# Attention, gated MLP and routed experts on one core: VectorE's row transpose moved into a PSUM bank, and another order of the first expert tiles while the last chunk is routed

## What is computed

```python
scores = scale * q @ k.T, causal window of 64, softmax        # 4 x 8 heads, 576 positions, 64 wide
x = attention output as 2304 tokens x 512
xn = x / rms(x) * rms_g
x = (silu(xn @ w_gate) * (xn @ w_val)) @ w_out                # 512 -> 1536 -> 512
logits = x @ w_gate2;  noisy = logits + log1p(exp(x @ w_noise)) * noise   # 8 experts
top-2 experts per token, softmax weights over the two
out[token] += weight * (relu(x[token] @ w1[e]) @ w2[e])       # 512 -> 1024 -> 512
```

## Time and profile before

| | |
|---|---|
| median of three executions | 1112.79 us (1111.0 to 1114.4) |
| profiled execution, its own time | 1109.55 us |
| its span, first to last instruction | 1107.7 us |
| mean granted TensorE clock | 0.995 |
| TensorE matmul busy | 1076.5 us, 97% of the span |
| VectorE busy | 587.5 us, 53% |
| ScalarE busy | 324.2 us, 29% |
| GpSimd busy | 404.6 us, 37% |

### The profile page before, as it was taken

One profiled execution on the slowest core, in us unless ns is written; L12 is line 12 of the kernel. 1 busy time (PEld: TensorE's weight loads), 2 busy tenths in 40 slices (PEclk: granted clock), 3 DMA queues, 4 the chain that ended last, 5 costly groups with the idle time before them and its releaser, 6 DMA issues.

```text
span 1107.7 us, 20151 instructions
## 1 busy us (share of the span) xinstructions
PE 1076.5 (97%) x6113; PEld 940.3 (85%) x6114; DVE 587.5 (53%) x1209; ACT 324.2 (29%) x712; POOL 404.6 (37%) x370
## 2 busy tenths in 40 slices
PE   8999999999999999999998899999999999999995
PEld 7878999999998999999986788888888888888884
DVE  6777334353352353453447767565655666565551
ACT  7996122332431432432353002030302020110241
POOL 3557992022022022010187107070706142331485
PEclk9999999999999999999999999999999999999998
DMA  7975527013013022010185427171625353332675
GB/s 213 270 243 194 171 86 276 1 58 114 1 59 115 1 74 80 5 54 1 46 245 172 110 48 199 38 199 47 179 65 153 78 134 110 99 90 52 172 231 190
DMA packets 167356, 129.40 MB, mean 117 GB/s; under 512 B 96720, under 2 KB 128864, under 8 KB 167296
## 3 DMA queue, kind: packets, MB, share of 16 engines
q1 hardware_dynamic: 145440, 71.20, 22.9%
q10 hardware_dynamic: 16032, 38.47, 11.0%
q0 software_dynamic: 5824, 18.95, 5.1%
HBM read 85.87 MB, written 42.73 MB: 116 GB/s over the span
## 4 chain that ended last, share of the span: by engine, by line
PE 87%; POOL 4%; issue 3%; DMA 2%; DVE 2%; ACT 1%; SPq 0%; POOLq 0%; ACTq 0%; DVEq 0%
PE bank L792 26%; PE bank L953 18%; PE bank L969 18%; PE bank L824 13%; PE bank L982 3%; PE bank L738 3%; PE bank L765 2%; POOL token_rows_a L679 1%; PE bank L748 1%; PE bank L732 1%; PE bank L860 1%; DMA token_rows_b<-expert_rows,slots_u 1%; POOL token_rows_a L692 1%; ACT p_sb L1102 1%; PE bank L871 1%
## 5 line engine op out<-in xcount | busy, mean ns | idle before, releaser
L792 PE MATMUL bank<-x_parts,mlp_weights 128*128 128x384 f32 x1704 | 311.9, 337 | 0.4 <-issue 0.4
L792 PEld LDWEIGHTS bank<-x_parts,mlp_weights 128*128 128x128 f32 x1704 | 296.9, 188 | 6.1 <-issue 0.8
L953 PE MATMUL bank<-expert_parts,xT_high 128*128 (+1 forms) x688 | 217.2, 397 | 6.2 <-DVE xT_low L1640 5.4
L969 PE MATMUL bank<-expert_parts,hT_high 128*128 (+1 forms) x688 | 212.0, 389 | 1.5 <-DVE hT_low L1651 1.5
L663 POOL TENSOR_TENSOR expert_parts<-raw_expert_a,expert_parts 128x512 fp32r<-128x512 f32 x64 | 82.1, 1315 | 243.9 <-ACT expert_parts L1249 243.9
L824 PE MATMUL bank<-mlp_weights,hidden_parts 128*128 128x512 f32 x648 | 162.2, 394 | 1.1 <-ACT y_sb L1173 1.1
L953 PEld LDWEIGHTS bank<-expert_parts,xT_high 128*128 128x128 f32 x688 | 126.6, 189 | 31.4 <-issue 4.7
L969 PEld LDWEIGHTS bank<-expert_parts,hT_high 128*128 128x128 f32 x688 | 129.0, 188 | 28.3 <-issue 1.7
L824 PEld LDWEIGHTS bank<-mlp_weights,hidden_parts 128*128 128x128 f32 x648 | 120.0, 188 | 24.9 <-ACT y_sb L1173 1.4
L953 PE MATMUL bank<-expert_parts,xT_low 128*128 (+1 forms) x344 | 134.8, 392 | 0.0
L969 PE MATMUL bank<-expert_parts,hT_low 128*128 (+1 forms) x344 | 134.1, 390 | 0.0
(11 more groups left out here) (204 smaller groups left out, 1238.6 us busy)
## 6 DMA issues: line engine op xcount, KB each, us to landing
raw_expert_a<-in_w ACTq DMA_DIRECT2D x32, 512.0 KB, 4.0
raw_expert_b<-in_w ACTq DMA_DIRECT2D x32, 512.0 KB, 4.4
x_row<-routed_rows SPq DMA_DIRECT2D x172, 64.0 KB, 2.6
expert_rows<-y_row SPq DMA_DIRECT2D x43, 256.0 KB, 2.0
expert_rows<-zeros SPq DMA_DIRECT2D x4, 2304.0 KB, 13.0
v_sb<-in_v SPq DMA_DIRECT2D x32, 256.0 KB, 3.6
q_sb<-in_qT SPq DMA_DIRECT2D x16, 288.0 KB, 3.7
k_sb<-in_kT SPq DMA_DIRECT2D x16, 288.0 KB, 4.2
```

Of the source, the lines that this page charges most:

```text
L792: last = nc.tensor.matmul(bank[:, 0:CHUNK], w_sb[:, i, wp, at:at + P], xp[:, par, part, k, :], start=n == 0, stop=n == 3 * KB - 1)
L953: last = nc.tensor.matmul(ps[half][:, 0:512], (xTh, xTl)[xp][:, k, :], ew_sb[:, bass.ds(slot, 1), wp, k * F2 + half * 512:k * F2 + half * ...
L969: last = nc.tensor.matmul(ps[5][:, 0:D], (hTh, hTl)[hp][:, f, :], ew_sb[:, bass.ds(slot, 1), 2 + wp, f * D:(f + 1) * D].rearrange("p a n - ...
```

## The change

It has two parts. First, `x_T` is no longer an SBUF tensor but bank 6 of PSUM, for all 43 tiles, so the block transpose writes PSUM, and the rounded copy and the subtraction read PSUM. Second, the opening order changes. On TensorE, the logits product of the last chunk goes between the two halves of the k loop of tile 0's second up half; tile 1's first up half goes ahead of `pe_hT(0)`; the counts and ranks go into the middle of tile 1's second up half; `pe_hT(1)` and tile 2's first up half go ahead of the table's rows. On VectorE, `dve_xT` is cut in three, and its parts for tile 1 stand around the copies of the logits; ReLU of tile 0's second half comes after them; `dve_top2` comes ahead of `dve_hT(0)`, and `dve_slots` stands between the two halves of `dve_hT(0)`, ahead of ReLU of tile 1.

```diff
--- before.py
+++ after.py
@@ -195,7 +195,6 @@
     assert moe.pos - keep.pos <= KB * CHUNK * 8
     xTh = moe.take("xT_high", [P, KB, P], F32R)
     xTl = moe.take("xT_low", [P, KB, P], F32R)
-    x_T = moe.take("x_transposed", [P, KB, P], F32)
     relu = moe.take("relu", [P, F2], F32)
     hTh = moe.take("hT_high", [P, FB2, P], F32R)
     hTl = moe.take("hT_low", [P, FB2, P], F32R)
@@ -940,7 +939,8 @@
             mlp_loop(pe, pe_chunk)
             pe_down(pe, CHUNKS - 1, FB - 1)
 
-        def pe_up2(pe, t, slot, expert, halves=(0, 1)):
+        def pe_up2(pe, t, slot, expert, halves=(0, 1), between=None):
+
             pe.wait_ge(xTl_done, t + 1)
 
             pe.wait_ge(expert_low, 16 * expert + 8)
@@ -949,6 +949,8 @@
                     pe.wait_ge(relu_done, 2 * t - 1 + half)
                 n = 0
                 for k in range(KB):
+                    if between and half == halves[-1] and k == KB // 2:
+                        between()
                     for wp, xp in PRODUCTS:
                         last = nc.tensor.matmul(ps[half][:, 0:512], (xTh, xTl)[xp][:, k, :],
                                                 ew_sb[:, bass.ds(slot, 1), wp, k * F2 + half * 512:k * F2 + half * 512 + 512].rearrange("p a n -> p (a n)"),
@@ -990,19 +992,22 @@
             pe_up2(pe, 0, 0, 0, (0,))
             for t in range(CHUNK_TILES):
                 pe_yT(pe, c, t)
-            pe_up2(pe, 0, 0, 0, (1,))
-            pe_logitsT(pe, c)
+            pe_up2(pe, 0, 0, 0, (1,), lambda: pe_logitsT(pe, c))
             pe_logits(pe, c)
+            pe_up2(pe, 1, 0, 0, (0,))
             pe_hT(pe, 0)
-            pe_up2(pe, 1, 0, 0)
-            pe.wait_ge(chosen_done, CHUNKS)
-            pe_chunk_counts(pe)
-            pe_count(pe, counted)
-            pe_ranks(pe, c)
+
+            def ranks():
+                pe.wait_ge(chosen_done, CHUNKS)
+                pe_chunk_counts(pe)
+                pe_count(pe, counted)
+                pe_ranks(pe, c)
+            pe_up2(pe, 1, 0, 0, (1,), ranks)
             pe_down2(pe, 0, 0, 0)
+            pe_hT(pe, 1)
+            pe_up2(pe, 2, 0, 0, (0,))
             pe_table_rows(pe)
-            pe_hT(pe, 1)
-            pe_up2(pe, 2, 0, 0)
+            pe_up2(pe, 2, 0, 0, (1,))
             pe_down2(pe, 1, 0, 0)
             pe.wait_ge(table_done, 1)
 
@@ -1625,22 +1630,33 @@
             nc.vector.tensor_tensor(kept[:, 1, :], kept[:, 1, :], swapped[:, 1, :], ALU.add
                                     ).then_inc(places, 1)
 
-        def dve_xT(dve, t, buf, earlier):
+        x_T = BANK_A[:].rearrange("p (k t) -> p k t", k=KB)
+
+        def dve_xT_turn(dve, t, buf, earlier):
 
             dve.wait_ge(x_row_in[buf], 16 * BLOCKS * earlier + 16 * BLOCKS)
             if not (isinstance(t, int) and t == 0):
                 dve.wait_ge(xTl_done, t)
-            nc.vector.transpose(x_T[:].rearrange("p k t -> p (k t)"), x_row[:, buf, :]).then_inc(xT_done, 1)
+            nc.vector.transpose(BANK_A[:], x_row[:, buf, :]).then_inc(xT_done, 1)
+
+        def dve_xT_high(dve, t):
             if not (isinstance(t, int) and t == 0):
 
                 dve.wait_ge(up_done, 2 * t)
             dve.wait_ge(xT_done, t + 1)
-            nc.vector.tensor_copy(xTh[:], x_T[:]).then_inc(xTh_done, 1)
+            nc.vector.tensor_copy(xTh[:], x_T).then_inc(xTh_done, 1)
+
+        def dve_xT_low(dve, t):
             dve.wait_ge(xTh_done, t + 1)
-            nc.vector.tensor_tensor(xTl[:], x_T[:], xTh[:].bitcast(F32), ALU.subtract).then_inc(xTl_done, 1)
-
-        def dve_hT(dve, t):
-            for b in range(2):
+            nc.vector.tensor_tensor(xTl[:], x_T, xTh[:].bitcast(F32), ALU.subtract).then_inc(xTl_done, 1)
+
+        def dve_xT(dve, t, buf, earlier):
+            dve_xT_turn(dve, t, buf, earlier)
+            dve_xT_high(dve, t)
+            dve_xT_low(dve, t)
+
+        def dve_hT(dve, t, halves=(0, 1)):
+            for b in halves:
                 dve.wait_ge(hT_done, 2 * t + b + 1)
                 if b == 0 and not (isinstance(t, int) and t == 0):
 
@@ -1673,14 +1689,17 @@
             dve_relu(dve, 0, (0,))
             for t in range(CHUNK_TILES):
                 dve_yT(dve, c, t)
+            dve_xT_turn(dve, 1, 1, 0)
+            dve_logitsT(dve, c)
+            dve_xT_high(dve, 1)
+            dve_logits(dve, c)
+            dve_xT_low(dve, 1)
             dve_relu(dve, 0, (1,))
-            dve_logitsT(dve, c)
-            dve_xT(dve, 1, 1, 0)
-            dve_logits(dve, c)
-            dve_hT(dve, 0)
             dve_top2(dve, c)
+            dve_hT(dve, 0, (0,))
+            dve_slots(dve, c)
+            dve_hT(dve, 0, (1,))
             dve_relu(dve, 1)
-            dve_slots(dve, c)
             dve_xT(dve, 2, 0, 1)
             link = dve_table(dve)
             dve_y(dve, 0)
```

## The result

The changed kernel takes 1117.04 us (median of 8 executions, 1115.68 to 1118.89), the kernel before 1112.01 us (8 executions, 1111.0 to 1114.4). The ratio is 1.0042, with a 95% interval of 1.0029 to 1.0055: slower by 0.42%, where 1110.6 us, a little faster, was forecast. Its profiled execution took 1117.85 us, with a span of 1116.0 us.

The account below looks back on a forecast made before the run. TensorE bounds the repeating pattern; in the opening, the chain to tile 3's rows decides. Loads 1.29 us earlier plus 0.86 from tile 3's chain make 2.15 off 1112.79: 1110.6 us, range 1107.0 to 1113.6.

Parts of the forecast that it names:

- Part 1, the table: VectorE's table behind the slots: 3.6 us to its columns at 600.6, table_done at 602.1 against 600.46 before.
- a gain for tile 3: Bank operands avoid the collision with GpSimd, so tile 3's three-operation chain takes 2.21 us, 0.86 less.
- SP passes its waits: SP waits for scatter and table before loading tile 3's rows: at 602.05 against 603.34, 1.29 us earlier.
- The landing: Tile 3's four row loads and their landing after SP passes: 8.64 us, taken as unchanged.
- ScalarE as the gate: Last chunk's softplus: its function table load stands behind expert weights, so Exp starts at 585.25 earliest, Ln ends at 587.0.
- the late table as what comes next: After the softplus gate, the table could be late next: table_done at 602.1, falling together with the scatter.
- The bank: PSUM for x_T in all tiles: transpose 0.70 us, copy 0.68, subtraction 0.69, repeating pattern unchanged.
- The slower one: Rival: transpose into a bank as slow as the reciprocal, 2.7 us more; 3.9 us slower, 1116.7; chance 0.05.
- the 2.7 us of my forecast: TensorE's idle time before tile 3's up product: about 2.7 us against 3.25, with the slow clock behind it kept.
- my rival on the clock: Clock stays up behind the shorter idle time before tile 3: 1.59 us more gain, 1109.0; chance 0.21.

Follow-up runs that it names:

- table_one_input: Changed kernel with the table's products reading one input from bank 6 and its last operation using two scalars: 1116.61 us, ratio 1.0029 to the kernel before.
- softplus_first: split_after_table with ScalarE computing the last chunk's softplus ahead of the copy of weight piece 10: 1109.72 us, ratio 0.9976 to the kernel before.
- bank_only: Kernel before with the transpose going into the PSUM bank and the old order kept: 1111.15 us, ratio 0.9991 to the kernel before.
- probe_small: bank_only plus one VectorE operation per tile, 8 elements wide with two SBUF inputs: 1118.19 us, one run.
- split_after_table: Changed kernel with GpSimd waiting for table_done before splitting the first pair's last five pieces: 1111.49 us, ratio 0.9992 to the kernel before.

## Why the prediction was wrong

**The step that failed** is the one headed "Part 1, the table", where I wrote "then the table: 3.6 us up to its columns". It took 610.30 - 598.98 = 11.3 us. I took the 3.6 from a stretch in which GpSimd issued indirect stores, and moved the table by my own sum to 597.0 to 600.6 and its last copies to 602.1, right up to the start of GpSimd's splits (601.6 before), without asking what else reads SBUF there. My own sum moved the splits as well: they start when the stores are issued, 8.2 us behind the slots before, so with slots at 592.12 at 600.3, before the table's columns at 600.6. I had the collision in hand, as the earlier trace rows shows it for the wide operations, and used it only as a gain for tile 3. The table's operations are of the same kind. table_one_input shows that even a table whose products are through in time is caught, by one of its small steps.

**The sum, in distances from the MLP's end** (573.30 in the forecast, 575.19 measured):

| step | forecast | measured |
|---|---|---|
| Ln of the softplus ends | 13.7 | 13.7 |
| slots written | 18.8 | 19.0 (before: 20.1) |
| table begins | 23.7 | 23.8 |
| SP passes its waits | 28.8 | 36.5 |
| rows landed | 37.4 | 45.8 |
| tile 3's up product | 40.0 | 48.5 |

The start of the table is right within 0.2 us; the next line is 7.7 off, which is the 7.8 us of `at_row` above its usual 0.17. The landing took 9.3 us from SP's passing where I let 8.64 stand, 0.7 more: it is no constant, but shared with the weights' loads, 2.51 to 6.38 us for the last of four in the runs above. That term was mis-sized in the forecast as well.

**ScalarE as the gate** was right, and so was the late table as what comes next; its size was not. softplus_first shows what lies behind the gate: `dve_top2` comes into GpSimd's splits itself, where it took 5.5 us in place of 3.2.

**The bank** was right in all its terms: the transpose 0.716 us where I took 0.70, the copy 0.69 without a value above, the subtraction 0.69 without one of 1.6, tile 3's chain 621.01 to 623.26, 2.25 us where I had 2.21. The pattern is unchanged at full TensorE. bank_only alone ended 1.0 us under before by the ratio, near the 0.86 of that term, though the interval does not tell it from nothing.

**The rivals.** The slower one came out near in time (1116.7 against 1117.04) by chance, and wrong in mechanism: the transpose is not slow. The rival that counted was missing. Of the clock: the idle time before tile 3 was 1.10 us, and the up product behind it took 5.73 us, at the high level; but TensorE ran at the low one behind two new stalls, in tile 1's and tile 2's second halves (matmuls of 0.63 us at 593.25 and 611.76, granted clock 0.54 from 592.10 to 594.60 and 0.56 from 610.30 to 617.00), off the path. For idle time like the 2.7 us of my forecast, probe_small has 2.73 us before tile 3 and an up product of 7.34 us behind it, bank_only 2.24 and 7.28: there the slow clock stood, as I had let it stand. But split_after_table has 2.84, and the matmuls behind it (0.40 us from 615.97 on) ran at the high level: the length of this idle time does not decide it alone, and my rival on the clock stays open.

## What to carry to other kernels

Before a block of small VectorE operations is moved, lay GpSimd's timeline beside the place it moves to. A duration read under one neighbour does not hold under another, and a two-input operation of 8 columns can be shut out for a whole run of GpSimd's two-input operations. Moving a block earlier can bring it into another such run, as softplus_first shows. Where the order can't avoid it, hold GpSimd's work with a wait until the small block, and the transfers that TensorE waits for, are through. Together with ScalarE's softplus moved ahead of one weight copy, that turned the same change from 0.42% slower to 0.48% faster; in the kernel before the wait alone changed nothing.

## What the runs showed of the hardware beyond the forecast

- The lock-out lasts for a run of GpSimd's operations, not for one: 7.98, 8.06, 8.05, 7.82 and 8.16 us behind six splits in five profiles, 5.77 in a sixth, where the operation asked when the run was under way. It ended each time within 0.1 us of the run's end, and it was gone in split_after_table, where the run was held back. Other operations, wide ones above all, were let in at the first border; the rule between them is open.
- In those five profiles the operation that was hit asked 0.33 to 0.54 us into the last indirect store, before the first split is on record. Operations with two SBUF inputs that asked earlier in the same store ran at once: `is_at` of the changed kernel, 0.26 us into it, took 0.15 us.
- A GpSimd memset of 8 columns between the splits did not let the waiting operation in (8.16 us).
- The same down product took 5.60 us a tile in the two kernels that shift its SBUF inputs by 320 or 32 bytes a partition, and 5.45 in the twelve others; whether the shift is the cause was not tested.
- VectorE's block transpose writes a PSUM bank at nearly the speed of SBUF: 716 against 701 ns for 128x512.
